# A gated recurrent attention layer and two expert layers: the products with the values split over the two column halves of TensorE

## The chip, the cores and the metric

The kernel runs on one core of a Trainium2 chip. The metric is the device time of one execution in microseconds, taken as the median over runs. TensorE is called PE below, and its weight load PEld; VectorE is DVE, ScalarE ACT, GpSimd POOL, and SyncE (which only issues DMAs here) SP.

## The reference, cut to what matters

There are two batches of 8 heads, 768 tokens and 40 features per head. A recurrent attention (an mLSTM) runs over the tokens, and its result goes through two expert layers (`moe` and `moe2`, each two wide products with a gate and one product back).

```
for t in range(S):
    m_new = np.maximum(f_gate[:, :, t] + m, i_gate[:, :, t])
    f_stab = np.exp(f_gate[:, :, t] + m - m_new)
    i_stab = np.exp(i_gate[:, :, t] - m_new)
    C = f_stab * C + i_stab * einsum('bhd,bhe->bhde', vt, kt)
    n = f_stab * n + i_stab * kt
    h_tilde = einsum('bhde,bhe->bhd', C, qt)
    denom = max(abs(n . qt), 1)
    y[:, :, t] = sigmoid(o_gate) * h_tilde / denom
x = y as [1536, 320]
x = (sigmoid(x @ w_gate) * (x @ w_val)) @ w_out
x = rms_norm(x) * rms_g
out = (silu(x @ w_gate2) * (x @ w_val2)) @ w_out2
```

## The kernel before, in words

The recurrence is computed in chunks of 128 tokens. There are 12 chunks, numbered n = 0 to 11: batch b = n % 2, place in the sequence j = n // 2. Each chunk is a list of pieces, and each engine has its own part of a piece:

- D: PE makes the log weights for all 8 heads (L929 and L931 for the first two chunks, L936 for the others), and ACT takes their exponential (L553) into `wexp`, 128 source tokens by 8 heads by 128 target tokens. In memory `wexp` is the tensor `tail`.
- S: PE multiplies keys and queries (L954). A head has 40 features, so two heads go at once, one on the array's rows 0 to 63 and one on its rows 64 to 127. DVE multiplies the result into `wexp` in two halves of 4 heads (L753), and each half counts up `p_done`.
- N: PE multiplies the carried state with the queries (L969, chunks 2 and up) and then `wexp` with the values (L977). L977 is the line that changes. It has one product per head: `wexp[b][:, h, :]`, 128 by 128, is loaded as weights, and the 41 columns of the head's values (40 and a column of ones) stream past. All 8 heads write side by side into one PSUM bank, on 128 partitions, one partition per target token. The last one counts up `n_done`. DVE then combines and divides (L762 to L781; the last of these counts up `y_done`).
- K: PE makes the chunk's own contribution to the state (L987); DVE and POOL add it (L788, L792, L474, L477).
- T: PE transposes the result for the expert layers (L895), ACT and DVE write it as a high and a low part (`x_hi` L587, `x_lo` L808). R is a small piece for decay factors (L945, L946, L575, L576).

The pieces D, S, N, K, T of chunks 0 and 1 come first, then D of chunk 2 and R. All others are woven by hand, in the table `WEAVE`, between the products of the first expert layer, which runs for 4 blocks of two chunks each: 12 slots with the two wide products (`hidden`, L1026, L1027, L1029: 16 matmuls of 256 columns per slot) and 4 slots with the product back (`project`, L1093 to L1095). In the rest of the kernel, the second half, the remaining tokens go through both layers in groups of 512 (`hidden_pair`, L1077, and `project`), and no chunk of the recurrence is left.

PE works in program order. The first `hidden` waits for `x_done` of both first chunks and for the first split weights. Every weight chunk is loaded by SP's queue into one of three buffers, rounded to a high part on ACT (L538, L543) and given its low part on POOL (L436, L441, L450), which frees its buffer; `split0` counts these. `hidden` waits for two more of them every third slot, and `project` for one more every third step.

PE's matmuls of plain fp32 data (L954, L977, L987, L969) have two records in the profile for each one in the program. L977 has 96 in the program and 192 records.

Of the kernel before, what the change touches and what calls it, by code (L numbers as in the profile page):

```python
# [17 lines left out]
D1 = D + 1  # L18
# [25 lines left out]
HALF = P // 2  # L44
# [27 lines left out]
def mlstm_moe_kernel(nc, gates, qk_t, q_t, vok, w_gv, w_o, rms_g, out):  # L72
# [5 lines left out]
    with ctx:  # L78
# [74 lines left out]
        wexp = [t[:, 0:H * P].rearrange("p (h t) -> p h t", t=P) for t in tails]  # L153
# [3 lines left out]
        va = [t[:, QK + QT:QK + QT + HE] for t in step]  # L157
# [28 lines left out]
        bank = [ctx.enter_context(nc.psum_tensor(f"bank{i}", [P, 512], F32)) for i in range(8)]  # L186
# [4 lines left out]
        def base(n):  # L191
            return 0 if n == 1 else 4

        def kv_bank(n):
            return bank[(3, 1)[n]] if n < 2 else bank[4]
# [39 lines left out]
        def o_bank(n):  # L235

            if n < M0 - B:
                return bank[7]
            return bank[n - (M0 - B)] if n < NT - B else bank[4 + n - (NT - B)]

        def part_of(j):
            return [j0 <= j < j1 for j0, j1 in PARTS].index(True)

        def y_slot(n):
            return 1 if n == 1 else 0
# [646 lines left out]
        def _(pe):  # L892
            def turn(ps, s):
                for c in range(3):
                    mm = pe.transpose(t_view(ps)[:, c, :], y_tok[:, s, c * P:(c + 1) * P], ident[:, :])  # L895
                return mm

            def seven(what):

                kind, n, *_ = IN_SEVEN[IN_SEVEN.index(what) - 1] if what != IN_SEVEN[0] else ("", 0)  # L900
                if kind == "N":
                    pe.wait_ge(num_done, n - B + 1)
                elif kind == "R":
                    pe.wait_ge(r_exp, n)
                elif kind == "O":
                    pe.wait_ge(x2_done, n + 1)

            def piece(what):
                kind, n, *_ = what
                b = n % B  # L910
                j = n // B
                if kind == "D":
                    if n < B:
                        pe.wait_ge(drhs_done, n + 1)
                        pe.wait_ge(selc_done, n + 1)
                        pe.wait_ge(consts, 2)
                    else:
                        pe.wait_ge(fill_done, 3)
                        pe.wait_ge(lhs_done, part_of(j))
                        pe.wait_ge(flat_in, 32 * j)  # L920

                        if n > B:
                            pe.wait_ge(cn_done, min(n, NT - B))
                        pe.wait_ge(p_done, 2 * n)
                    for i in range(2):
                        dp = bank[base(n) + i]
                        r0 = H * b + 4 * i
                        if j == 0:
                            pe.matmul(dp[:, :], ident_b[:, :], causal[:, :].unsqueeze(1).to_broadcast([P, 4, P]),  # L929
                                      start=True, stop=False)  # L930
                            mm = pe.matmul(dp[:, :], d_lhs0, d_rhs0[:, r0:r0 + 4, :].rearrange("p q t -> p (q t)"),  # L931
                                           start=False, stop=True)
                        else:
                            for u in range(2):
                                us = slice(HALF * u, HALF * u + HALF)
                                mm = pe.matmul(dp[:, :].rearrange("p (q t) -> p q t", t=P)[:, :, us],  # L936
                                               d_lhs[:, j - 1, u, :], d_rhs[:, r0:r0 + 4, us], start=True, stop=True)
                        mm.then_inc(d_done, 1)
                elif kind == "R":
                    j0, j1 = PARTS[n]  # L940
                    rv = bank[7][:, 0:2 * NJ * R].rearrange("p (w j r) -> p w j r", w=2, r=R)
                    pe.wait_ge(lend_done, n)
                    seven(what)
                    for jj in range(j0, j1):
                        pe.transpose(rv[:, 0, jj, :], l_r[:, jj * P:(jj + 1) * P], ident[0:R, 0:R])  # L945
                    pe.matmul(rv[:, 1, j0:j1, :], ones[:, :], l_end[:, j0:j1, :, :].rearrange("p j b h -> p j (b h)"),  # L946
                              start=True, stop=True).then_inc(r_mm, 1)
                elif kind == "S":
                    pe.wait_ge(qk_in[b], 32 * (j + 1))
                    pe.wait_ge(e_done, 2 * n + 2)  # L950
                    for c in range(4):
                        for i in range(2):
                            rs = slice(64 * i, 64 * i + D)
                            mm = pe.matmul(bank[base(n) + i][:, c * P:(c + 1) * P], sq[b][rs, 1, c, :], sq[b][rs, 0, c, :],  # L954
                                           start=True, stop=True)
                            if c == 3:
                                mm.then_inc(s_done, 1)
                elif kind == "N":
                    if j:
                        pe.wait_ge(q_in[b], 16 * j)  # L960
                        if j == 1:
                            pe.wait_ge(cn_done, b + 1)
                        else:
                            pe.wait_ge(cst_done, n - 2 * B + 1)
                        pe.wait_ge(r_exp, part_of(j))
                        seven(what)
                        for g in range(NG):
                            cs = slice(g * GH * D1, min((g + 1) * GH, H) * D1)
                            pe.matmul(bank[7][:, cs], q3[b][0:KR, g, :], cst[b][:, cs], start=True, stop=True)  # L969
                    if n >= B:  # L970
                        pe.wait_ge(x_done, n)
                    pe.wait_ge(vo_in[b], 16 * (j + 1))
                    for i in range(2):
                        pe.wait_ge(p_done, 2 * n + i + 1)
                        for c in range(4):
                            h = 4 * i + c
                            mm = pe.matmul(bank[base(n) + 2][:, h * D1:(h + 1) * D1], wexp[b][:, h, :],  # L977
                                           va[b][:, h * D1:(h + 1) * D1], start=True, stop=True)
                    mm.then_inc(n_done, 1)
                elif kind == "K":  # L980
                    pe.wait_ge(kn_in[b], 16 * (j + 1))
                    pe.wait_ge(vk_done, n + 1)

                    pe.wait_ge(p_done, 2 * B if n < B else 2 * n + 1)
                    for g in range(NG):
                        cs = slice(g * GH * D1, min((g + 1) * GH, H) * D1)
                        mm = pe.matmul(kv_bank(n)[0:KR, cs], kn[b][:, g * KR:(g + 1) * KR], vk[b][:, cs],  # L987
                                       start=True, stop=True)
                    mm.then_inc(k_done, 1)
                elif kind == "T":  # L990
                    pe.wait_ge(y_done, n + 1)
                    turn(bank[base(n) + 2], y_slot(n)).then_inc(t_done, 1)
                elif kind == "O":
                    pe.wait_ge(yo_done, n + 1)
                    if n < M0 - B:
                        seven(what)
                    else:

                        pe.wait_ge(hf_done, F2 if n < NT - B else F2 + NF)
                    turn(o_bank(n), 1 + n % B).then_inc(ot_done, 1)  # L1000
# [103 lines left out]
            for kind in "DSNKT":  # L1104
                for n in range(B):
                    piece((kind, n))
            piece(("D", 2))
            piece(("R", 1))
            for k in range(NB0):
                for slot in range(NF + 4):  # L1110
# [77 lines left out]
```

## Time and profile before

| | |
|---|---|
| median of 3 runs | 470.79 us (470.5 to 472.61) |
| the profiled execution, its own time | 472.79 us |
| its span in the profile | 471.0 us |
| PE busy | 463.7 us (98%) |
| PE weight loads busy | 424.3 us (90%) |
| DVE, ACT, POOL busy | 225.9, 192.8, 109.6 us |
| granted clock of TensorE, mean | 0.986 |

The own time of the profiled execution has 1.79 us beside the span. Records of matmuls overlap: one lasts longer than the distance to the next, so the cost of a group is read from starts (from the first start of the group to the first start of what follows it), not from the mean of a record. A clock of 1.00 in the profile's windows is 2.4 GHz and one of 0.50 is 1.2 GHz.

### The profile page before, as it was taken

How to read it: one execution, taken by the hardware profiler on the slowest of the kernel's cores; microseconds unless marked ns; L12 is line 12 of the kernel's file. 1: busy time of each engine (PE TensorE's matmuls, PEld its weight loads, DVE VectorE, ACT ScalarE, POOL GpSimd, SP SyncE). 2: the span in 40 equal slices, each digit the busy share in tenths (PEclk: the TensorE clock that was granted, in tenths of full speed). 3: DMA queues.
4: the chain of work that ended last, by engine and by line, in shares of the span. 5: the costliest groups of instructions: out<-in, count | busy, mean ns of one | idle time of the engine just before them, and what ended most of it. 6: DMA issues, size and time to landing. Idle time of an engine off the chain costs nothing. (4 is left out here: it accounts for less than half of the span.)

```text
span 471.0 us, 9044 instructions
## 1 busy us (share of the span) xinstructions
PE 463.7 (98%) x3731; PEld 424.3 (90%) x3731; DVE 225.9 (48%) x455; ACT 192.8 (41%) x359; POOL 109.6 (23%) x148
## 2 busy tenths in 40 slices
PE   8999999999999999999999999999999999999997
PEld 3999999999999999998888988889988889888897
DVE  8747784684564545542344223664024570065520
ACT  8686628444638534621456233233113230123310
POOL 5969921211210220000475627000000000000000
PEclk9679999999999999999999999999999999999999
DMA  7555631112212220400132301000000000000001
GB/s 265 197 201 153 173 104 29 60 46 73 68 40 72 61 60 1 150 1 2 29 128 98 125 1 44 0 1 15 28 16 1 1 1 28 29 1 1 1 21 36
DMA packets 11471, 27.86 MB, mean 59 GB/s; under 512 B 1526, under 2 KB 5830, under 8 KB 11430
## 3 DMA queue, kind: packets, MB, share of 16 engines
q1 hardware_dynamic: 11110, 27.20, 18.1%
q8 instruction: 29, 0.48, 0.4%
q10 hardware_dynamic: 320, 0.08, 0.1%
q14 instruction: 12, 0.10, 0.1%
HBM read 25.23 MB, written 1.97 MB: 58 GB/s over the span
## 5 line engine op out<-in xcount | busy, mean ns | idle before, releaser
L626 ACT ACTIVATE sg<-bank 128x256 f32<-128x256 f32 (+1 forms) x96 | 47.1, 491 | 153.3 <-PE bank L1077 100.9
L1077 PE MATMUL bank<-x_hi,wgv_hi 64*128 64x512 f32 x576 | 105.9, 388 | 0.8 <-DVE x_lo L812 0.8
L1077 PE MATMUL bank<-x_lo,wgv_hi 64*128 64x512 f32 x480 | 93.9, 386 | 0.0
L849 DVE TENSOR_TENSOR hf<-sg,bank 128x256 f32<-128x256 f32 (+1 forms) x96 | 53.1, 553 | 70.3 <-ACT sg L626 68.1
L1026 PE MATMUL bank<-x_hi,wgv_hi 128*128 128x256 f32 x288 | 81.9, 293 | 0.0
L1027 PE MATMUL bank<-x_lo,wgv_hi 128*128 128x256 f32 x288 | 79.5, 285 | 0.0
L1093 PE MATMUL bank<-wo_hi,h_hi 128*128 128x320 f32 x240 | 75.5, 314 | 0.0
L1077 PE MATMUL bank<-x_hi,wgv_lo 64*128 64x512 f32 x384 | 75.1, 386 | 0.0
L1095 PE MATMUL bank<-wo_hi,h_lo 128*128 128x320 f32 x240 | 74.2, 309 | 0.0
L1094 PE MATMUL bank<-wo_lo,h_hi 128*128 128x320 f32 x240 | 74.1, 309 | 0.0
L847 DVE TENSOR_TENSOR sg<-sg,bank 128x512 f32<-128x512 f32 x36 | 24.8, 688 | 87.4 <-ACT sg L626 85.4
L1077 PEld LDWEIGHTS bank<-x_hi,wgv_hi 64*128 64x128 f32 x576 | 54.4, 184 | 12.7 <-DVE x_lo L812 1.2
L1026 PEld LDWEIGHTS bank<-x_hi,wgv_hi 128*128 128x128 f32 x288 | 56.0, 194 | 0.7
L1027 PEld LDWEIGHTS bank<-x_lo,wgv_hi 128*128 128x128 f32 x288 | 56.0, 194 | 0.0
L1029 PE MATMUL bank<-x_hi,wgv_lo 128*128 128x256 f32 x192 | 54.8, 285 | 0.0
L1077 PEld LDWEIGHTS bank<-x_lo,wgv_hi 64*128 64x128 f32 x480 | 45.3, 184 | 8.9
L853 DVE TENSOR_TENSOR h_lo<-hf,h_hi 128x256 fp32r<-128x256 f32 (+1 forms) x84 | 48.7, 579 | 0.1
L1093 PEld LDWEIGHTS bank<-wo_hi,h_hi 128*128 128x128 f32 x240 | 45.1, 188 | 1.4 <-issue 1.1
L1094 PEld LDWEIGHTS bank<-wo_lo,h_hi 128*128 128x128 f32 x240 | 45.1, 188 | 0.0
L1095 PEld LDWEIGHTS bank<-wo_hi,h_lo 128*128 128x128 f32 x240 | 45.1, 188 | 0.0
L632 ACT ACTIVATE h_hi<-hf 128x256 fp32r<-128x256 f32 (+1 forms) x84 | 42.3, 504 | 4.4 <-DVE hf L849 4.4
L1077 PEld LDWEIGHTS bank<-x_hi,wgv_lo 64*128 64x128 f32 x384 | 36.3, 184 | 7.3
(131 smaller groups left out, 614.3 us busy)
## 6 DMA issues: line engine op xcount, KB each, us to landing
step<-in_vok SPq DMA_DIRECT2D x12, 324.0 KB, 3.0
step<-in_qk_t SPq DMA_DIRECT2D x24, 160.0 KB
step<-in_w_gv SPq DMA_DIRECT2D x6, 576.0 KB, 3.7
raw_p<-in_w_gv SPq DMA_DIRECT2D x5, 576.0 KB, 4.4
raw_x<-in_w_gv SPq DMA_DIRECT2D x5, 576.0 KB, 5.2
step<-in_vok SPq DMA_DIRECT2D x10, 180.0 KB, 3.7
step<-in_q_t SPq DMA_DIRECT2D x10, 180.0 KB, 3.3
raw_x<-in_w_o SPq DMA_DIRECT2D x3, 480.0 KB, 3.4
```

What stands on the lines that cost most here:

```text
L626: act.activation(sg_view(n), g_view(n), ACT.Sigmoid).then_inc(sg_done, 1)
L632: act.activation(h_view(n, 0), hf_view(n), ACT.Copy).then_inc(hhi_done, 1)
L847: dve.tensor_tensor(sg_view(n), sg_view(n), g_view(n), ALU.mult).then_inc(silu_done, 1)
L849: dve.tensor_tensor(hf_view(n), sg_view(n), v_view(n), ALU.mult).then_inc(hf_done, 1)
L853: dve.tensor_tensor(h_view(n, 1), hf_view(n), h_view(n, 0).bitcast(F32), ALU.subtract).then_inc(h_done, 1)
L1026: pe.matmul(ps, wgv_hi[:, wc, s, cs], x_hi[:, xs, s, :], start=(s == 0), stop=False)
L1027: mm = pe.matmul(ps, wgv_hi[:, wc, s, cs], x_lo[:, xs, s, :], start=False, stop=(s == 2))
L1029: pe.matmul(ps, wgv_lo[:, wc, s, cs], x_hi[:, xs, s, :], start=False, stop=False)
L1077: mm = pe.matmul(ps(n), w, x, start=own and (s, p) == (0, 0), stop=last and not own)
L1093: pe.matmul(ps, h_view(n0 + f, 0)[:, ts], wo_hi[:, f, :], start=(f == 0), stop=False)
L1094: pe.matmul(ps, h_view(n0 + f, 0)[:, ts], wo_lo[:, f, :], start=False, stop=False)
L1095: mm = pe.matmul(ps, h_view(n0 + f, 1)[:, ts], wo_hi[:, f, :], start=False, stop=(f == NF - 1))
```

## The change

Each of the 8 products of a chunk becomes two: one with the weights' first 64 columns (target tokens 0 to 63), which writes PSUM partitions 0 to 63, and one with the other 64 columns, which writes partitions 64 to 127. Both stream the same 41 columns of values. Order, waits and counts stay as they are; the last of the 16 matmuls counts up `n_done`.

```
                         for c in range(4):
                             h = 4 * i + c
-                            mm = pe.matmul(bank[base(n) + 2][:, h * D1:(h + 1) * D1], wexp[b][:, h, :],
-                                           va[b][:, h * D1:(h + 1) * D1], start=True, stop=True)
+
+                            for u in range(2):
+                                us = slice(HALF * u, HALF * u + HALF)
+                                mm = pe.matmul(bank[base(n) + 2][us, h * D1:(h + 1) * D1], wexp[b][:, h, us],
+                                               va[b][:, h * D1:(h + 1) * D1], start=True, stop=True)
                     mm.then_inc(n_done, 1)
```

`HALF` is 64 and `D1` is 41.

## Rows read from the trace of the kernel before

**Rows 1.** The page: busy time, and the 40 slices of the span.
```profile
PE 463.7 (98%) x3731; PEld 424.3 (90%) x3731; DVE 225.9 (48%) x455; ACT 192.8 (41%) x359; POOL 109.6 (23%) x148
PEclk9679999999999999999999999999999999999999
```
**Rows 2.** Who waited for whom, PE: us in total, times, longest.
```profile
PE bank L895 <- DVE x_lo L812: 1.0, 2, 0.7
PE bank L977 <- DVE tail L753: 0.8, 1, 0.8
PE bank L1077 <- DVE x_lo L812: 0.8, 1, 0.8
```
**Rows 3.** Groups by form, PE and PEld: busy us, mean ns.
```profile
L977 PE MATMUL bank<-step,tail 128*128 128x41 f32 x192 | 25.1, 296 | 0.8 <-DVE tail L753 0.8
L977 PEld LDWEIGHTS bank<-step,tail 128*128 128x128 f32 x192 | 24.5, 208 | 1.0 <-issue 1.0
```
**Rows 4.** Timeline of PE, chunk 3: start us, us, what.
```profile
51.75 0.28 PE L1026 MATMUL bank<-x_hi,wgv_hi 128*128 128x256 f32 x1
51.87 0.28 PE L1027 MATMUL bank<-x_lo,wgv_hi 128*128 128x256 f32 x1
51.99 0.76 PE L987 MATMUL bank<-tail,step 128*120 128x123 f32 x6
52.59 0.83 PE L969 MATMUL bank<-cst,step 120*128 120x123 f32 x6
53.26 1.92 PE L977 MATMUL bank<-step,tail 128*128 128x41 f32 x16
55.01 0.36 PE L1026 MATMUL bank<-x_hi,wgv_hi 128*128 128x256 f32 x1
55.21 0.28 PE L1027 MATMUL bank<-x_lo,wgv_hi 128*128 128x256 f32 x1
```
**Rows 5.** Timeline of PE around the S piece of chunk 4, same columns.
```profile
76.75 0.28 PE L1026 MATMUL bank<-x_hi,wgv_hi 128*128 128x256 f32 x1
76.88 0.28 PE L1027 MATMUL bank<-x_lo,wgv_hi 128*128 128x256 f32 x1
77.08 1.16 PE L954 MATMUL bank<-step 40*128 40x128 f32 x16
78.18 0.39 PE L1026 MATMUL bank<-x_hi,wgv_hi 128*128 128x256 f32 x1
78.40 0.28 PE L1027 MATMUL bank<-x_lo,wgv_hi 128*128 128x256 f32 x1
```
**Rows 6.** The same piece in three short windows, up to 77.19, 77.31, 77.42.
```profile
77.08 0.38 PE L954 MATMUL bank<-step 40*128 40x128 f32 x2
...
77.08 0.49 PE L954 MATMUL bank<-step 40*128 40x128 f32 x4
...
77.08 0.60 PE L954 MATMUL bank<-step 40*128 40x128 f32 x6
```
**Rows 7.** Timeline of PE at the start, chunks 0 and 1.
```profile
13.54 6.00 PE L977 MATMUL bank<-step,tail 128*128 128x41 f32 x32 [0.81 <-DVE tail L753]
19.33 2.71 PE L987 MATMUL bank<-tail,step 128*120 128x123 f32 x12
21.83 1.49 PE L895 MATMUL bank<-ident,y_tok 128*128 128x128 f32 x6
22.97 1.20 PE L936 MATMUL bank<-d_rhs,d_lhs 128*128 128x256 f32 x4
```
**Rows 8.** Timeline of DVE in the same stretch.
```profile
13.32 1.86 DVE L753 TENSOR_TENSOR tail<-bank,tail 128x512 f32<-128x512 f32 x3
16.15 0.17 DVE L767 TENSOR_SCALAR den<-bank 128x8 f32<-128x8 f32 x1 [0.97 <-PE bank L977]
17.71 0.88 DVE L781 COPY y_tok<-y_tok 128x64 f32<-128x64 f32 x1
19.57 0.17 DVE L767 TENSOR_SCALAR den<-bank 128x8 f32<-128x8 f32 x1 [0.97 <-PE bank L977]
21.13 0.87 DVE L781 COPY y_tok<-y_tok 128x64 f32<-128x64 f32 x1
```
**Rows 9.** Windows: us, busy by engine, PEclk (the value behind the brackets), DMA.
```profile
14.66:24.75 10.09, 10.09 (x50) 9.83 (x49) 6.55 (x16) 5.44 (x7) 8.93 (x9) 0.50 0.58 198
24.75:28.30 3.55, 3.55 (x17) 3.55 (x17) 0.50 (x2) 3.43 (x8) 0.41 (x1) 0.50 0.72 233
28.30:30.30 2.00, 2.00 (x18) 1.89 (x16) 0.42 (x1) 1.99 (x3) 1.92 (x3) 1.00 0.00 0
```
**Rows 10.** Timelines of POOL (weight splits) and PE (the last split's user).
```profile
19.57 0.99 POOL L441 TENSOR_TENSOR wgv_hi<-raw_x,wgv_hi 64x384 fp32r<-64x384 f32 x1
...
58.10 2.99 POOL L450 TENSOR_TENSOR wo_lo<-raw_x,wo_hi 128x320 fp32r<-128x320 f32 x3
...
62.88 0.31 PE L1093 MATMUL bank<-wo_hi,h_hi 128*128 128x320 f32 x1
```

## The prediction

> **What bounds the kernel now.** I read the page first. PE is busy for 98% of the span, in nearly every slice, and no other engine comes near [rows 1]. The waits that PE itself has sum to a few microseconds of 471 [rows 2]. So the kernel is bound by the order of work on PE, and time taken off a piece on PE comes off the end, unless PE then arrives somewhere before its data. Next the groups: the line that changes has 192 records of matmuls and 192 of loads, 25 us as busy time [rows 3]. Busy time is no cost here, since records overlap, so I read the cost from starts in the timeline. A warm N piece runs from 53.26 to the next product at 55.01: 1.75 us for 16 records, 0.109 us each [rows 4]. Ten chunks (2 to 11) are like that. The first two chunks together take 13.54 to 19.33, 5.79 us for 32 records [rows 7], most of it at a granted clock of 0.50, which is 1.2 GHz [rows 9].
>
> What sets the 0.109 us? Not the stream: the state's product next to it streams 123 columns instead of 41 and takes (53.26 - 52.59) / 6 = 0.112 us. It also loads 128 columns of weights. The one before, L987, loads 120 and streams 123, and takes (52.59 - 51.99) / 6 = 0.100 us [rows 4]. So an N record costs the load of its 128 columns; the 41 columns of values are hidden under the next load. That is what the change can halve: each load now has 64 columns.
>
> **The change part by part.**
>
> (1) *More instructions.* A chunk's 16 records of 128 columns become 32 of 64 columns. If time goes with loaded columns, one costs about 0.109 / 2 = 0.055 us plus a fixed share. From 112 ns at 128 columns and about 0.105 at 120 (the 0.100 above is a mean that holds a short first step) I take 5 ns fixed, so 0.058 us. Alone, in a row, 32 of them are 1.87 us, no gain.
>
> (2) *Side by side.* No row of before has two products on different columns. The nearest is the S piece, which has two products on different rows. The window up to 77.19 holds two records that start within 0.01 us of each other (each lasts some 0.37, the two together 0.38), and then every 0.11 us two more come [rows 6]. So a pair of loads of 128 columns on disjoint rows takes the time of one. If disjoint columns behave like that, a pair of N takes the time of one load of 64 columns, 0.058 us, and 16 pairs 0.93 us. The bounds of a pair are 0.055 (both together, no fixed share) and 0.117 (one after the other). I take 0.058, since the S rows are the nearest of their kind.
>
> Here a rule can be weighed that speaks against the change. The trace shows loads that run under a matmul on the same rows: N's distance of 0.109 us is that of a load alone, though each matmul record lasts 0.296 [rows 3, 4]. The Trainium skill says, in TensorE: Matmul & The Clock Gate, under "The mechanism", that weight loads overlap with matmuls in flight only when the row groups differ, or go to the background weights. The two halves of N use the same 128 rows. By that rule's strict side the second half's load would wait for the first half, and there would be no gain; TensorEngine Tiling, under "Key Properties", says on the other hand that different tiles load and multiply in parallel. No row settles it for columns.
>
> (3) *Issue.* In S, two loads and two matmuls go every 0.11 us, 28 ns an instruction. N would need four in 0.058 us, 15 ns an instruction. The trace shows starts closer than that inside a pair, but no row shows such a rate kept up over 64 instructions. The upper bound from the S row is 0.11 us per pair, which is nearly the serial case again.
>
> (4) *Going into the split array and out of it.* S pays for it. Its first start comes 0.20 us after the product before it, where 0.12 is the usual distance: 0.08. Its 8 pairs run to the next product in 1.10 us, where 8 times 0.11 is 0.90: 0.20. The product after comes 0.22 later instead of 0.12, but after N it is 0.20 already, so 0.02 new [rows 4, 5]. Together 0.30 us for each N, and I take the same for columns. Its lower bound is nothing, its upper bound about twice S's if both sides drain fully.
>
> (5) *A warm chunk.* 16 x 0.058 + 0.30 = 1.23 us instead of 1.75: 0.52 us less. Ten chunks: 5.2 us.
>
> (6) *The start.* DVE's weighting of the four halves ends near 13.95, 14.6 and 15.18 (three ends of the 1.86 us block; each 0.62) [rows 8]. The second half of chunk 1's products can't begin before 15.2. They have 8 pairs, at half clock about 0.117 each, 0.94 us, and some 0.2 of filling: chunk 1 ends near 16.4 rather than 19.33. K follows with its 2.50 us, to 18.9 [rows 7]. But T of chunk 1 needs `y_done`, which DVE gives 2.43 us after each chunk's L767 (16.15 to 18.59, 19.57 to 22.00) [rows 8]. DVE is free at 15.2; two of these, one after the other, end at 20.05. So T of chunk 1 starts near 20.1 instead of 22.4 (half way through L895's 21.83 to 22.97): 2.3 us less, of which DVE keeps back the other 0.6. D, R and the first `hidden` then move up, from 24.75 to about 22.4. The weights that it waits for are split at 20.56 [rows 10]. If the pairs are serial, the start gains nothing.
>
> (7) *The clock.* It is at 0.50 from 14.66 to 28.30 and rises 3.55 us after the first `hidden` began; 17 records take those 3.55 us, where 2.00 us hold 18 records at 1.00 [rows 9]. If the rise follows the earlier start of the dense work, nothing is added. If it still comes at 28.3, some 2.3 us more are run at 1.2 GHz, and 0.209 us per product against 0.12 loses 2.3 x (1 - 0.12 / 0.209) = 1.0 us. I take 0, and 0 to 1.0 as bounds.
>
> (8) *Nothing else moves.* DVE, ACT and POOL instructions are the same in number and size. DVE waits for N's end, not N for DVE, so an earlier `n_done` costs nobody. The other cover that could be gone is the weights: POOL's chain of splits in the first block ends at 61.09 and PE uses the last of them at 62.88 [rows 10], a margin of 1.8 us. Two warm N pieces lie between, 1.0 us, while the rest of POOL's chain moves up with the start. The margin holds; if the start moves and the chain doesn't, 0.5 to 1.5 us of PE wait appear once.
>
> Sum: 5.2 + 2.3 = 7.5 us, and 0 from the clock. The profiled execution took 472.79 us (471.0 span and 1.8 around it), 2.0 above the median: 465.3 for it. Against the median that is 470.8 - 7.5 = 463.3 us, 1.6% less. From the median this kernel can tell about 0.5% (2.35 us) from no change.
>
> **The rivals.**
>
> *Halves in pairs (the forecast)*, 463.3 us, own range 460 (no cost of going in and out of the split array, pair 0.055: 10 x 0.87 + 2.3) to 466 (the clock's 1.0, and that cost half as large again: 10 x 0.37 + 2.3 - 1.0). For it: the S rows. Chance 0.58.
>
> *Serial loads.* The two halves of one head are loaded one after the other. Then a chunk takes 32 x 0.058 + 0.30 = 2.16 us, 0.41 more than 1.75; ten chunks 4.1 us, the start 0.6 more for its doubled fixed shares and switching: 475.5 us, slower. The place is every N piece; the point from which it decides is the pair distance (1.75 - 0.30) / 16 = 0.091 us: above it each warm N loses. For it: both halves read the same 128 partitions and use the same rows, unlike S. Against it: loads already run under matmuls on the same rows. Chance 0.19. This is what the first rule of the Trainium skill in (2), from TensorE: Matmul & The Clock Gate, would make of the time.
>
> *Issue in between.* Pairs go together, but no faster than some 0.085 us: 16 x 0.085 + 0.30 = 1.66, 0.09 less per chunk, 0.9 in all, and about 1.5 at the start: 468.4 us. Chance 0.12.
>
> *A wait takes the place of part of it.* The warm gain is real, but the weights' chain or the clock takes back the start's 2.3 us and more: 470.8 - 5.2 + 1 = 466.6 us. Chance 0.05.
>
> *No overlap, or no narrower load.* If a load of 64 columns costs as much as one of 128 and they don't pair, 32 x 0.112 + 0.30 = 3.88 us, 2.1 more per chunk, 21 in ten, and some 5 at the start: 497 us. A load that also waits for the matmul before it ends near that. The load of 120 columns being cheaper than that of 128 speaks against it. Chance 0.06.
>
> **How the numbers follow.** The likeliest case gives 463.3. Its own range is 460 to 466. The forecast, the wait and the in-between case hold 0.75; to reach 0.8 the serial case must be in, so the range is 460 to 475.5. Faster by over 0.5% (below 468.4): 0.58 + 0.05 + half of the in-between 0.12, 0.69. Within 0.5%: the other half and the mild end of the serial case, 0.08. Slower: 0.23.
>
> **What the profile after would show.** L977 with 384 records and loads of 128 by 64. In a warm chunk, starts in pairs within 0.01 us, pairs 0.055 to 0.06 apart, and 1.2 us from the first to the next `hidden`. About 0.2 before the first pair. At the start, L977 over by 16.4, L895 of chunk 1 near 20.1, the first `hidden` near 22.4, DVE's idle time before L767 gone. Distances of 0.058 from record to record without pairs would show the serial case; pairs 0.08 or more apart, issue; a new wait of PE on L441 or L450 the weights. The prediction fails if column halves don't pair as row halves do, or if switching costs more than 0.8 us a chunk, which eats the gain.

## The result and the profile after

The changed kernel takes 464.74 us as the median of 4 runs (464.64 to 465.01), the kernel before 471.01 us (470.5 to 472.61). The ratio is 0.9862, interval 0.9838 to 0.9886: 1.4% faster, 6.3 us. The forecast was 463.3 us, 7.5 us less. The profiled execution took 464.66 us, of which the span is 462.9.

The page: PE is still the bound, and has 192 more matmuls.

```profile
PE 452.5 (98%) x3923; PEld 410.1 (89%) x3923; DVE 227.0 (49%) x455; ACT 193.1 (42%) x359; POOL 109.8 (24%) x148
PEclk9999999999999999999999999999999999999999
```

Timeline of PE around chunk 3 (start us, us, engine, line, what), the piece of [rows 4]. The lines of the kernel have moved down by 3 behind the change, so L980 is the changed product, L990 and L1029 are L987 and L1026 of before:

```profile
48.82 0.83 PE L969 MATMUL bank<-cst,step 120*128 120x123 f32 x6
49.59 1.13 PE L980 MATMUL bank<-step,tail 128*64 128x41 f32 x32
50.65 0.39 PE L1029 MATMUL bank<-x_hi,wgv_hi 128*128 128x256 f32 x1
50.87 0.28 PE L1030 MATMUL bank<-x_lo,wgv_hi 128*128 128x256 f32 x1
```

Twice as many records (32), and from the first start to the next product 50.65 - 49.59 = 1.06 us instead of 1.75. The same piece in three short windows, up to 49.60, 49.76 and 49.81, as S was shown in [rows 6]:

```profile
49.59 0.26 PE L980 MATMUL bank<-step,tail 128*64 128x41 f32 x2
...
49.59 0.37 PE L980 MATMUL bank<-step,tail 128*64 128x41 f32 x6
...
49.59 0.43 PE L980 MATMUL bank<-step,tail 128*64 128x41 f32 x8
```

Two records are there from the first moment, and from six to eight, one pair more, the block grows by 0.06 us. The column halves behave like the row halves of S: a pair takes the time of one load of 64 columns. The last start is 49.59 + 1.13 - 0.23 (one record) = 50.49, 15 steps of 0.060 us in the mean: the first is 0.08, the others are 0.058.

The start, PE's timeline, beside [rows 7]:

```profile
13.54 2.37 PE L980 MATMUL bank<-step,tail 128*64 128x41 f32 x64 [0.81 <-DVE tail L753]
15.84 1.50 PE L990 MATMUL bank<-tail,step 128*120 128x123 f32 x12
17.60 0.55 PE L895 MATMUL bank<-ident,y_tok 128*128 128x128 f32 x3 [0.26 <-DVE y_tok L781]
19.93 0.55 PE L895 MATMUL bank<-ident,y_tok 128*128 128x128 f32 x3 [1.79 <-DVE y_tok L781]
21.66 0.58 PE L1029 MATMUL bank<-x_hi,wgv_hi 128*128 128x256 f32 x1 [0.31 <-DVE x_lo L808]
```

PE now waits 1.79 us for DVE before T of chunk 1, and the first hidden product starts at 21.66 instead of 24.75. The clock in windows (us, busy by engine, PEclk, DMA), beside [rows 9]:

```profile
14.66:21.55 6.89, 4.61 (x59) 3.91 (x57) 5.92 (x16) 5.08 (x7) 6.58 (x7) 1.00 0.42 139
21.55:24.97 3.42, 3.31 (x15) 3.32 (x16) 0.86 (x3) 3.30 (x8) 2.40 (x3) 0.50 0.86 305
```

The clock stays at its upper level (2.4 GHz) until 21.55. It falls for 3.42 us after PE's wait for DVE, just as the hidden products begin. A cover has become thin: in `project` of the first chunk, PE now uses POOL's last split 0.5 us after it is done (54.95 + 3.06 = 58.01, used at 58.55), where [rows 10] had 1.8 us.

```profile
54.95 3.06 POOL L450 TENSOR_TENSOR wo_lo<-raw_x,wo_hi 128x320 fp32r<-128x320 f32 x3
...
58.55 0.31 PE L1096 MATMUL bank<-wo_hi,h_hi 128*128 128x320 f32 x1
```

One wait is new against the first profile of before. There, the state product of chunk 4 (L969) had no row among PE's waits; now the view of waits has the second line below. The first is T at the start, as shown above:

```profile
PE bank L895 <- DVE y_tok L781: 2.0, 2, 1.8
PE bank L969 <- DVE x_lo L812: 0.7, 1, 0.7
```

### The profile page after: what moved, and what is told of

The parts are those of the page before. It is cut to its first block and busy times, and to the rows that moved or that the text cites. A ratio compares the mean times of both kernels' runs of the same rounds, so it can differ in the third digit from the quotient of the medians.

```text
span 462.9 us, 9428 instructions
## 1 busy us (share of the span) xinstructions
PE 452.5 (98%) x3923; PEld 410.1 (89%) x3923; DVE 227.0 (49%) x455; ACT 193.1 (42%) x359; POOL 109.8 (24%) x148
## 5 line engine op out<-in xcount | busy, mean ns | idle before, releaser
L1029 PE MATMUL bank<-x_hi,wgv_hi 128*128 128x256 f32 x288 | 81.9, 294 | 0.3 <-DVE x_lo L808 0.3
L1029 PEld LDWEIGHTS bank<-x_hi,wgv_hi 128*128 128x128 f32 x288 | 55.8, 194 | 1.5 <-DVE x_lo L808 0.4
L853 DVE TENSOR_TENSOR h_lo<-hf,h_hi 128x256 fp32r<-128x256 f32 (+1 forms) x84 | 50.4, 601 | 0.1
```

Source lines behind the costliest of these rows:

```text
L853: dve.tensor_tensor(h_view(n, 1), hf_view(n), h_view(n, 0).bitcast(F32), ALU.subtract).then_inc(h_done, 1)
L1029: pe.matmul(ps, wgv_hi[:, wc, s, cs], x_hi[:, xs, s, :], start=(s == 0), stop=False)
```

## The experiments

Beside the first four runs, the kernel before took 471.92 us.

**The same half first.** Within four heads, all products on columns 0 to 63, then all on 64 to 127.

```
-for c in range(4):
-    for u in range(2):
+for u in range(2):
+    for c in range(4):
```

> The same 16 half-width products per chunk as in the change, in another order: within each group of four heads first the four products on columns 0 to 63, then the four on columns 64 to 127. Theory (the gain comes from two loads on different column halves that stand next to each other): only one record in eight now has a neighbour on the other half, so records come one by one, about 0.058 us apart, a warm chunk takes about 32 x 0.058 + 0.2 = 2.05 us from its first start to the next product, 0.3 us more than before the change, and the whole is 473 to 476 us. Rival (a narrower load is enough, or PE finds the partner by itself further down its queue): 1.06 us a chunk as in the changed kernel and 464.7 us.

Measured: 467.5 us (467.38 to 468.79), ratio 0.9922 (0.9896 to 0.9948). PE's timeline around chunk 3, and the number of records in windows of 0.08 us (the value behind the second number):

```profile
49.74 1.44 PE L979 MATMUL bank<-step,tail 128*64 128x41 f32 x32
51.11 0.39 PE L1028 MATMUL bank<-x_hi,wgv_hi 128*128 128x256 f32 x1
...
49.90:49.98 0.08, 0.08 (x4) 1.00 1.11 384
50.10:50.18 0.08, 0.08 (x9) 1.00 0.87 336
50.36:50.44 0.08, 0.08 (x10) 1.00 0.54 208
```

A chunk takes 1.37 us, between the two theories. A record lasts 0.23 us; where they start singly every 0.058 us, a window of 0.08 holds about (0.23 + 0.08) / 0.058 = 5 of them, where pairs start about 10. It is 4 at the beginning and 9 or 10 around the places where one half's products end and the other's begin. So order counts (10 chunks x 0.31 = 3.1 us, and 2.8 us were lost against the change), narrower loads alone are not what gains, and both simple theories were wrong in part: PE doesn't need its partner to be the very next product. Short windows, all from 49.60 on and up to 49.99, 50.01, 50.19 and 50.25, show how it goes:

```profile
49.74 0.43 PE L979 MATMUL bank<-step,tail 128*64 128x41 f32 x4
49.74 0.51 PE L979 MATMUL bank<-step,tail 128*64 128x41 f32 x6
49.74 0.66 PE L979 MATMUL bank<-step,tail 128*64 128x41 f32 x11
49.74 0.69 PE L979 MATMUL bank<-step,tail 128*64 128x41 f32 x12
```

Four records start singly in the first 0.25 us, and seven in the next 0.20, two every 0.058 us. The 32 starts of the chunk fit four strings of eight, one for each half of each four heads, with 0.058 us from start to start inside a string (0.08 at its first step) and 0.26 us from the first start of one string to the first start of the next: 3 x 0.26 + 0.43 + 0.16 = 1.37 us. A string thus begins while the last three records of the one before it have yet to start. The records don't name their columns, so this is a reading, but it accounts for every start and for the 1.37 us. It also shows what one half costs by itself, 0.058 us for each load of 64 columns. Why the next string begins after 0.26 us and not at once isn't shown.

**Chunks 2 to 11 alone, and chunks 0 and 1 alone.**

```
-for u in range(2):
+parts = 2 if n >= B else 1      # the other run: 2 if n < B else 1
+for u in range(parts):
```

> The change for chunks 2 to 11 alone; chunks 0 and 1 keep the products of full width. Theory (ten warm chunks are worth 0.57 us each, the start is worth the rest): the gain over the kernel before is 5.7 us less the wait of 0.7 us that the changed kernel has at the state product of chunk 4, so 5.0 us, and the start still has a low clock for some 13 us. Rival (the start gives most of it): under 3 us of gain.

> The change for chunks 0 and 1 alone. Theory: the first hidden product starts about 3.1 us earlier than before, since the clock stays at its upper level over the products and the state product of the first two chunks, and the kernel gains that, less 1 us or more for a clock that is low a little later: 1 to 3 us. Rival (the clock at the start falls by chance and not for what PE does): the trace shows 0.50 from about 14.7 us on, as before the change, the first hidden product starts near 22.4, and the gain is about 2.3 us at most.

Measured: 467.86 us, ratio 0.9916 (0.9885 to 0.9946), 4.0 us, for chunks 2 to 11; 470.88 us, ratio 0.9976 (0.996 to 0.9993), 1.1 us, for the first two. The warm chunks are most of the gain. The 5.0 us expected lie inside the interval of the first run (2.5 to 5.4 us); its waits hold, beside the 0.7 us at chunk 4, 0.5 us for POOL's last split, which the expectation had not counted:

```profile
PE bank L1096 <- POOL wo_lo L450: 0.5, 1, 0.5
```

The start gives far less than the 2.7 us by which the first hidden product moved in its profile (24.75 to 22.03). The windows of that run show where a part goes:

```profile
14.66:20.73 6.07, 3.96 (x62) 3.43 (x59) 5.64 (x15) 4.94 (x7) 5.83 (x6) 1.00 0.57 170
20.73:27.56 6.83, 6.83 (x33) 6.57 (x33) 1.79 (x4) 6.66 (x11) 5.58 (x7) 0.50 0.77 265
```

The rival "by chance from 14.7 on" is out in this execution: the clock is up over the first chunks' products and low for 6.83 us after them, 5.5 of them over hidden products (from 22.03 on), where the first profile of before has 3.55. That leaves 1.8 of the 2.7 us (spans of 469.2 and 471.0). The rest is no loss: the first profile of before, with 472.79 us, is among that kernel's longest executions, as shown below.

**The gate scan later.** To find what the wait at chunk 4 hangs on.

```
-[("O", 0), ("A", 3, 0)], [("S", 4)], [("O", 1), ("A", 3, 1)], [K, N], [("Y", 4)], [("D", 5)],
+[("O", 0)], [("S", 4)], [("O", 1)], [K, N], [("Y", 4), ("A", 3, 0)], [("D", 5), ("A", 3, 1)],
```

> The changed kernel with the first two DVE steps of the last gate scan moved from slots 1 and 3 to slots 5 and 6 of the second block. Theory (the new wait of PE at chunk 4's state product, 1.0 us between starts instead of 0.3 before the change and 0.1 elsewhere, comes from DVE being late with x_lo of chunk 1 of the second layer, because the scan stands ahead of it): the wait goes, the distance falls to 0.1 to 0.3 us, and the kernel is 0.7 to 0.9 us faster than the changed one, about 463.9. Rival (the wait hangs on ACT or on the norm before it): no change, 464.7.

Measured: 463.84 us (463.74 to 465.08), ratio 0.9841 (0.9812 to 0.9871). PE's timeline at chunk 4 in the changed kernel, then in this one:

```profile
78.12 0.77 PE L990 MATMUL bank<-tail,step 128*120 128x123 f32 x6
79.63 0.87 PE L969 MATMUL bank<-cst,step 120*128 120x123 f32 x6 [0.74 <-DVE x_lo L812]
```

```profile
78.09 0.77 PE L990 MATMUL bank<-tail,step 128*120 128x123 f32 x6
78.69 0.83 PE L969 MATMUL bank<-cst,step 120*128 120x123 f32 x6
```

The wait is gone, so the scan ahead of `x_lo` was its cause, and the time is 0.9 us lower than the change's median, as the theory had it. The intervals of the two ratios overlap. The two profiles also differ at the start: in this one the granted clock is at 1.00 throughout, so chunk 2's N begins 1.2 us earlier than in the changed kernel's (32.30 and 33.51), and PE then waits for POOL instead:

```profile
PE bank L1096 <- POOL wo_lo L450: 0.6, 1, 0.6
```

The fair neighbour is the run with idle matmuls below, whose profile has the same clock and the same wait on POOL, and the wait at chunk 4 besides: 464.38 us against 463.74, so 0.6 us for the wait.

Beside the next runs, the kernel before took 470.61 us.

**Quarters.**

```
-for u in range(2):
-    us = slice(HALF * u, HALF * u + HALF)
+for u in range(4):
+    us = slice(32 * u, 32 * u + 32)
```

> Each product with the values split into four of 32 weight columns each, in neighbouring order, instead of two of 64. Theory (a group of neighbouring records takes the time of one load, about 5 ns and 0.83 ns a column, 58 ns measured for 64 columns): four records every 32 to 40 ns, a warm chunk 0.75 to 0.8 us from its first start to the next product instead of 1.06, and 2 to 3 us less than the changed kernel, 462 us. Rival (the 58 ns are a floor of issue for four instructions, or the stream of the 41 columns): four records every 58 to 117 ns, 1.06 to 2.0 us a chunk, and 465 to 474 us.

Measured: 463.64 us (462.79 to 463.66), ratio 0.9844 (0.9822 to 0.9865), with the change itself at 464.83 beside it. PE's timeline:

```profile
51.39 0.82 PE L980 MATMUL bank<-step,tail 128*32 128x41 f32 x64
52.14 0.39 PE L1029 MATMUL bank<-x_hi,wgv_hi 128*128 128x256 f32 x1
```

0.75 us for 64 records: groups of four about 0.62 / 16 = 0.039 us apart. No floor of issue or of the stream stood at 0.058. The whole gains only 1.2 of the 3.1 us that ten chunks have. Most of the rest is lost at the start, as PE's timeline there shows:

```profile
18.59 0.55 PE L895 MATMUL bank<-ident,y_tok 128*128 128x128 f32 x3 [1.43 <-DVE y_tok L781]
23.25 0.58 PE L1029 MATMUL bank<-x_hi,wgv_hi 128*128 128x256 f32 x1
```

T of chunk 0 starts 1.0 us later than in the changed kernel (17.60), since DVE's steps before it took longer (its L779 1.18 us instead of 0.49), D and R then run at the low clock, and the first hidden product starts 1.6 us later (21.66 there). The clock was at 0.50 for 4.5 us of hidden products, against 3.3 to 3.4 in the change's profiles, some 0.5 us more. Why DVE was slower isn't shown; a later run with quarters (the second of the last three) has its first hidden product at 21.65.

**Every other head split.** Eight changes between the split and the full array in a chunk instead of two, to see what a change costs.

```
+parts = 2 if n < B or c % 2 == 0 else 1
```

> In chunks 2 to 11 only every other head's product is split into halves, the others have full width, so that PE changes between the two shapes eight times a chunk instead of twice. Theory (each change costs by itself: 0.09 us more before the first pair and 0.1 us more after the last one): a split head and a full one take 0.205 + 0.08 + 0.16 + 0.11 = 0.56 us, a chunk 2.2 us instead of 1.06 with all heads split and 1.74 with none, and the whole comes out at 475 to 477 us, slower than before the change. Rival (the 0.3 us of a chunk are paid once for the piece): 8 pairs of 0.058 and 8 records of 0.112 and 0.3, 1.66 us, about 470 us.

Measured: 476.09 us, ratio 1.0111 (1.0077 to 1.0145).

```profile
51.90 2.44 PE L980 MATMUL bank<-step,tail 128*64 128x41 f32 x24
54.17 0.36 PE L1029 MATMUL bank<-x_hi,wgv_hi 128*128 128x256 f32 x1
```

2.27 us a chunk, against 2.2 expected and 1.66 of the rival. Each change of shape costs by itself. Of a chunk's 2.27 us, 4 x (2 x 0.058 + 2 x 0.112) = 1.36 are loads, and 0.9 are the seven changes inside the stretch, 0.13 us each. The eighth lies before the first pair: 0.21 us after L969's last start instead of 0.11.

**The kernel before and the change, once more.**

> The kernel before, profiled once more. Theory (the clock at the start of the kernel before is low for a time that differs from one execution to the next, and mostly lies on the products and state products of the first two chunks): another length of the stretch at 0.50 than 13.6 us, the time per record of those pieces changes with it, and every warm chunk again takes 1.744 us. Rival: the same stretch from 14.7 to 28.3 us.

> The changed kernel once more, beside the others of this group. Theory: 464.7 us again, ratio 0.986; one stretch of 3.4 us at 0.50 near the first hidden products, or none. Rival (the first result was helped by the clock's luck at the start): 466 us or more.

Measured: the kernel before 470.01 us, the change 464.83 us (464.8 to 464.84), ratio 0.9873 (0.985 to 0.9897). The kernel before, PE's timeline at the start and a window:

```profile
13.54 4.00 PE L977 MATMUL bank<-step,tail 128*128 128x41 f32 x32 [0.17 <-DVE tail L753]
17.33 2.71 PE L987 MATMUL bank<-tail,step 128*120 128x123 f32 x12
22.67 0.39 PE L1026 MATMUL bank<-x_hi,wgv_hi 128*128 128x256 f32 x1 [0.31 <-DVE x_lo L808]
...
16.86:20.28 3.42, 3.42 (x19) 3.42 (x18) 3.25 (x8) 2.02 (x2) 3.26 (x4) 0.50 0.53 172
```

Here the low stretch is 3.42 us, not 13.6, and the hidden products start at 22.67, not 24.75. The start of the kernel before is not one number: its runs with a mean clock of 0.996 took 470.0 to 470.4 us, those with 0.986 took 472.7 to 472.8. At a mean clock of 0.996 on both sides, the change (464.6 to 465.0 us) gains about 5.3 us.

Where the low stretch lies does go with the change, though. It begins at 14.66, 14.66 and 16.86 us, while PE is in the first two chunks' products, in the three profiles in which these have full width (both of the kernel before, and chunks 2 to 11 alone). In the eight in which they are split and PE has no idle matmuls, it begins between 20.2 and 22.4 us, or in one not at all. What makes the clock fall is not shown: in the split kernels PE has waited 1.79 us for DVE before it, but in the one that never falls it has waited as long.

And this execution of the kernel before has the wait at chunk 4 as well, 0.7 us on DVE's L812, in a kernel without the change. It comes where PE has gained on DVE in the first block: DVE's scan began 69.90 - 62.83 = 7.07 us ahead of PE's product L945 at the end of that block in the first profile of before and 66.44 - 60.06 = 6.38 us in this one, 0.69 us less. In all ten profiles that have the scan at its place and POOL's last split on POOL, the wait is what the lead lacks to 7.1 us: none at 7.07 (the first profile of before, and chunks 0 and 1 alone) and 7.26 (every other head), 0.4 at 6.70 (quarters), 0.55 at 6.56 (the same half first), 0.7 at 6.4 in the others. An earlier PE alone doesn't make it: with chunks 0 and 1 alone, chunk 3 came 1.8 us earlier than in the first profile of before, and the lead stayed. What shortens the lead isn't shown.

Beside the last four, the kernel before took 471.15 us.

**Idle matmuls at the start.**

```
+fill(7, 3) after S;  fill(0, 1) after K;  fill(0, 7) between the two T;  fill(0, 2) after R
+# fill(b, c): c matmuls of zeros, 128 x 512 bf16, into bank b
```

> The changed kernel with 13 idle matmuls (zeros, 128 by 512 bf16, into banks that nobody reads then) in the gaps that PE has before the first hidden products: 3 after S, 1 after K, 7 between the two T pieces, 2 after R. Theory (the low clock that meets the first hidden products comes from PE's wait for DVE before them, and what an earlier PE gains there is taken back by POOL's chain of weight splits at the end of the first block): no stretch at 0.50 from 14 to 28 us, the first 32 hidden products take 3.8 us instead of 5.4, a new PE wait of about 1 us for POOL's last split of the output weights appears, and the kernel gains 0 to 0.6 us, 464.2 to 464.8. Rival (nothing takes it back): 463.3 us.

Measured: 464.63 us (464.38 to 465.4), ratio 0.9856 (0.9832 to 0.9881). A window over the first hidden products, and a wait of PE:

```profile
21.64:25.67 4.03, 4.03 (x35) 3.90 (x33) 0.76 (x2) 3.91 (x8) 2.95 (x4) 1.00 0.89 299
...
PE bank L1096 <- POOL wo_lo L450: 0.6, 1, 0.6
```

The clock stays up, the first 32 hidden products and S of chunk 2 take 5.1 us (21.64 to 26.76) instead of 6.6 (21.66 to 28.21), and nearly nothing comes of it, since POOL's last split is now late: `project` of the first chunk runs from 53.14 to 59.62, 6.48 us, where the changed kernel has 54.59 to 59.89, 5.30. The 1.8 us of margin in [rows 10], of which the changed kernel had 0.5 left, are used up. The times of the changed kernel say the same: its four repeated runs have a mean clock of 1.0 once and of 0.995 or 0.996 three times, and all four took 464.80 to 464.84 us.

**All repairs, with halves and with quarters.** The idle matmuls, the later scan, and POOL's last split on DVE behind the gate scan of slot 12; then the same with quarters, without and with the idle matmuls.

```
-split(0, WCH - 1)                                   # POOL
+if k == 0 and slot == NF: dve.wait_ge(split0, WCH - 1); 3 x dve.tensor_tensor(wo_lo, raw, wo_hi, subtract)
```

> The changed kernel with three repairs: the idle matmuls at the start, the gate scan's first steps moved to slots 5 and 6 of the second block, and the last split of the first layer's output weights moved from POOL to DVE. Theory (PE's three waits or slow stretches each cost what they show: 1.5 us of low clock, 0.9 us at chunk 4, and about 1 us for POOL's last split once the others are gone): 464.8 - 1.5 - 0.9 = 462.4 us. Rival (DVE has no room for the split at the end of the first block): a new wait of PE on DVE there, and 463.5 us or more.

> Products with the values in quarters of 32 columns, the scan later and the last split on DVE, without the idle matmuls at the start. Theory (the 0.31 us per warm chunk that quarters save over halves come through once nobody else is late): 0.749 us per warm chunk, 0.1 us between the starts at chunk 4, 464.8 - 3.1 - 0.9 = 460.8 us with the clock at the start as in the changed kernel, up to 1.5 us more where it is low for longer. Rival (other engines take the place): waits of PE of more than 1 us in sum that the changed kernel doesn't have.

> The same with the idle matmuls at the start. Theory: the clock stays up over the first hidden products and the time is 459.5 to 460.5 us, about 2.3% less than the kernel before. Rival (POOL's and DVE's chains in the first block bound it now): the gain over the run without the idle matmuls is under 0.5 us.

Measured: 469.12 us (ratio 0.995, 0.9933 to 0.9967), 465.56 us (0.9883, 0.9852 to 0.9915) and 466.85 us (0.9902, 0.9874 to 0.993). All three medians are above the change's; the intervals of the second and third still overlap with that of the change. The wait of PE in the first and the place of the split in DVE's timeline:

```profile
PE bank L1105 <- DVE wo_lo L879: 4.3, 1, 4.3
...
59.27 0.73 DVE L718 TENSOR_TENSOR_SCAN l_r<-ones,f_r 16x128 f32<-16x128 f32 x2
59.93 0.39 DVE L719 TENSOR_TENSOR i_r<-i_r,m_r 16x256 f32<-16x256 f32 x1
60.35 1.30 DVE L879 TENSOR_TENSOR wo_lo<-raw_x,wo_hi 128x320 fp32r<-128x320 f32 x3
```

The rival held in all three (waits of 4.3, 3.5 and 4.3 us): DVE was 4 us late there with work of its own, and the split stood behind it. In the first and third, the clock fell during the wait, as the window in the first shows (us, busy by engine, PEclk, DMA):

```profile
61.16:67.99 6.83, 6.20 (x24) 6.19 (x25) 3.55 (x10) 0.91 (x3) 1.22 (x2) 0.50 0.00 0
```

So a wait can cost more than its own length: what PE does after it, up to 67.99, runs at 1.2 GHz. Whether a better place makes the repairs add up wasn't tried. The fastest versions measured are the change with the later scan (463.84) and quarters (463.64).

## Why the prediction was right

The mechanism was the forecast's likeliest, and each of its steps can be held against a number.

- *(1), (2) a load per pair.* Pair 0.058 us forecast, 0.058 to 0.060 measured. (The 0.105 us for a load of 120 columns was read rightly, but the short step in K is its last, not its first.) The serial case is refuted by the pairs in the short windows; with it goes the strict reading of the rule in TensorE: Matmul & The Clock Gate, which the Trainium skill gives under "The mechanism" for loads under matmuls on the same rows. The sentence of the Trainium skill, in TensorEngine Tiling under "Key Properties", that different tiles load and multiply in parallel agrees with the trace, with 0.06 us for two loads of 64 columns.
- *(3) issue.* No bound at 15 ns an instruction. Quarters went through at 0.039 us for eight, 5 ns each.
- *(4) in and out.* 0.30 us forecast. The first start comes 0.21 us behind L969's last instead of 0.11, so 0.09; inside, 1.06 - 0.93 = 0.13; behind, 0.02. That is 0.24. Splitting every other head shows that it is paid at each change, 0.13 us.
- *(5) a warm chunk.* 0.52 us forecast, 1.75 - 1.06 - 0.09 - 0.02 = 0.57 measured; ten make 5.7 against 5.2.
- *(6) the start.* This term was mis-sized: 2.3 us forecast, 1.1 us (0.3 to 1.9) measured with chunks 0 and 1 alone. Most steps inside it were right as times of the trace (the second T forecast near 20.1, measured 19.93; N forecast over at 16.4, measured 15.84, at full clock). But the sum took the one profiled execution as the kernel's start. That execution had a mean clock of 0.986, the lowest on record for this kernel, with the low stretch on those very pieces. Against it, the changed kernel's profile gains 3.1 us up to chunk 2's N (36.63 to 33.51), more than forecast. Against the other profile of before, in which this N starts at 33.00, it loses 0.5. The 1.1 us of the medians lie between.
- *(7) the clock.* Taken as zero, with 0 to 1.0 us as bounds. Against the first profile of before that was right: hidden products ran for 3.3 us at 0.50, where it had 3.55. Against the other, whose hidden products ran at full clock from the first one on, they pay for 3.3 us at 1.2 GHz, 3.3 x (1 - 0.12 / 0.209) = 1.4 us, beyond the bound.
- *(8) nothing else moves.* Wrong by 0.7 us. A wait at chunk 4 on DVE, with a cover that I hadn't looked for: the scan ahead of `x_lo` in DVE's queue. It is not made by the change as such, since the kernel before shows it in its other profile. The cover that I did name, POOL's splits with 1.8 us, held in the changed kernel with 0.5 us left. It was gone as soon as the clock stayed up, and also with chunks 2 to 11 alone, where PE waited 0.5 us for it.

The sum of what was measured is 5.7 - 0.7 + 1.1 = 6.1 us, against 6.3 between the medians. The two partial runs alone give 4.0 + 1.1 = 5.1 us, with intervals that hold the difference. The two profiles differ by 8.1 us in span (471.0 and 462.9), which is 3.1 + 5.7 - 0.7.

The total came out as near as it did in part by luck: the warm chunks were taken 0.5 us too low, the start 1.2 us too high, and the wait of 0.7 us at nothing. The first hides a part of the other two.

## What to carry to other kernels

Where loads of weights bound short matmuls (here plain fp32 with 41 streamed columns), split the weights over column halves, or quarters, and put the parts next to each other: a group takes the time of one narrow load, 0.058 us for 64 columns and 0.039 for 32, and about 0.24 us a piece goes to changing shape, so split whole runs of products and never every other one. Read a start stretch from more than one profile before its clock goes into a sum. And for every microsecond taken off the bound engine, list the next-latest chains with their margins over the whole stretch in which it gains, not only the one chain that feeds it.

## What the runs showed of the hardware that was not expected

- PE seems to start matmuls out of program order between column halves. With four heads of one half before four of the other, the starts fit strings of eight, each beginning while three records of the string before it have yet to start, and a chunk takes 1.37 us, not the 2.05 of strict order. "PE works in program order", as said above of the kernel, holds in this reading only among products on the same columns.
- Going from one array shape to another costs about 0.13 us each time for these products: seven changes 0.9 us with every other head split, and 0.24 us for the two of a chunk with all heads split.
- A group of neighbouring products takes 0.058 us for two of 64 columns and 0.039 for four of 32. In the second, 64 matmuls start within 0.62 us, one every 10 ns.
- The granted clock at the start of the same kernel was at 0.50 for 13.6 us in one execution and 3.4 us in another, and the time follows: 472.7 to 472.8 us with a mean of 0.986, 470.0 to 470.4 with 0.996. With thirteen idle matmuls in PE's gaps it was up in all 4 runs (mean 0.999 to 1.0). Without them it was at 1.0 in one run of the changed kernel and in one with the later scan.
